# Probabilities and values split into high and low parts, the row maxima sent as one row by DMA, and the dense block's weights split inside it

## What is computed

```python
# attention: 2 x 8 heads, 768 positions, 64 values each
q_bits = (q @ proj > 0); k_bits = (k @ proj > 0)     # 6 bits each: a bucket
mask = bucket(q)[:, None] == bucket(k)[None, :]
scores = where(mask, q @ k.T / 8, -1e9)
scores = scores - max(scores, axis=-1)
attn = exp(scores); attn = attn / (sum(attn) + 1e-9)
x = attn @ v                                         # (1536, 512) over the heads
# dense block
h = x @ w_in; g = where(h > 0, h, exp(min(h, 0)) - 1); y = g @ w_out   # 512 -> 2048 -> 512
# experts: rows with y @ w_skip > 0 go through one of 8 experts, chosen by y @ w_gate
```

## Time and profile before

| what | value |
|---|---|
| median of three runs | 715.51 us |
| profiled execution, span | 718.39 us, 716.5 us |
| first scores of head 0, first `up` of the dense block | 24.6, 295.1 us |
| PE busy | 678.6 us, 95% |
| DVE, ACT, POOL busy | 326.7, 238.2, 192.9 us |
| attention matmuls of `weighted` (L1125) | 384 records, 152.8 us |
| moved by DMA | 83.95 MB, mean 117 GB/s |

### The profile page before, as it was taken

The page is one execution under the profiler, slowest core; times in us unless marked ns, Lnnn a source line. Parts: engine busy times, 40 slices in busy tenths (PEclk is TensorE's granted clock), DMA queues, the critical chain, the costliest instruction groups (busy, mean ns, idle before and its releaser), DMA issues.

```text
span 716.5 us, 9192 instructions
## 1 busy us (share of the span) xinstructions
PE 678.6 (95%) x3472; PEld 574.7 (80%) x3472; DVE 326.7 (46%) x475; ACT 238.2 (33%) x365; POOL 192.9 (27%) x179
## 2 busy tenths in 40 slices
PE   4999999998999999999999999999998975999996
PEld 3677767676777777799999989989997954989995
DVE  6766656565666654133232223222314257446542
ACT  1233334333333334333342334233422321334330
POOL 3322253535162430659120002000002034112111
PEclk9999999999999999999999999999999995999999
DMA  7456656564555530412020002000366765699200
GB/s 176 118 129 141 165 125 163 125 162 96 139 117 133 116 89 10 131 44 67 1 90 1 1 0 88 0 0 0 146 200 206 241 238 188 237 346 334 89 11 24
DMA packets 69235, 83.95 MB, mean 117 GB/s; under 512 B 35540, under 2 KB 45780, under 8 KB 69200
## 3 DMA queue, kind: packets, MB, share of 16 engines
q1 hardware_dynamic: 67920, 79.83, 38.1%
q0 software_dynamic: 1280, 3.65, 1.6%
HBM read 56.64 MB, written 8.44 MB: 91 GB/s over the span
## 4 chain that ended last, share of the span: by engine, by line
PE 85%; DMA 5%; DVE 4%; SPq 2%; ACT 1%; issue 1%; POOL 0%; POOLq 0%; DVEq 0%; ACTq 0%
PE banks L1179 18%; PE banks L1166 18%; PE banks L1125 15%; PE banks L1290 8%; PE banks L1305 6%; PE banks L1093 5%; DMA k_hi_lo_T<-qk_lo_T 4%; PE banks L1112 4%; PE banks L1113 4%; SPq L312 2%; PE banks L1077 2%; PE banks L1197 1%; DVE g_lo L839 1%; PE banks L1101 1%; DVE row_max L770 1%
## 5 line engine op out<-in xcount | busy, mean ns | idle before, releaser
L1125 PE MATMUL banks<-probs,v_ones 128*128 128x384 f32 x384 | 152.8, 490 | 0.3 <-ACT o_and_den L629 0.3
L1166 PE MATMUL banks<-x_hi,w_split 128*128 (+1 forms) x512 | 142.4, 339 | 0.8 <-DVE g L860 0.8
L1179 PE MATMUL banks<-w_split,g_hi 128*128 128x512 f32 x384 | 122.2, 399 | 4.8 <-DVE g_lo L839 4.8
L860 DVE SCALAR_TENSOR_TENSOR g<-exp_min_h,banks 128x384 f32<-128x384 f32 x64 | 35.5, 554 | 198.0 <-ACT exp_min_h L672 197.8
L645 ACT ACTIVATE probs<-banks 128x768 f32<-128x768 f32 x96 | 77.8, 811 | 132.3 <-PE banks L1113 132.3
L770 DVE TENSOR_REDUCE row_max<-banks 128x1 f32<-128x768 f32 x96 | 91.4, 957 | 66.5 <-PE banks L1093 64.7
L1166 PEld LDWEIGHTS banks<-x_hi,w_split 128*128 128x128 f32 x512 | 94.2, 189 | 4.0 <-DVE g L860 1.1
L669 ACT ACTIVATE exp_min_h<-banks 128x384 f32<-128x384 f32 x64 | 31.5, 492 | 181.5 <-PE banks L1166 181.5
L1166 PE MATMUL banks<-x_lo,w_split 128*128 (+1 forms) x256 | 86.3, 337 | 0.0
L1179 PEld LDWEIGHTS banks<-w_split,g_hi 128*128 128x128 f32 x384 | 71.3, 190 | 18.0 <-DVE g_lo L839 6.0
L1093 PE MATMUL banks<-k_hi_rows_T,q_hi_rows_T 96*128 96x384 f32 x192 | 76.8, 487 | 7.8 <-DMA k_hi_lo_T<-qk_lo_T 7.5
(11 more groups left out here) (155 smaller groups left out, 835.0 us busy)
## 6 DMA issues: line engine op xcount, KB each, us to landing
expert_w<-in_moe_w SPq DMA_DIRECT2D x32, 1024.0 KB, 5.3
w_raw<-in_moe_w_in SPq DMA_DIRECT2D x16, 256.0 KB, 3.5
w_raw<-in_moe_w_out SPq DMA_DIRECT2D x16, 256.0 KB, 3.7
qk_nat<-in_q SPq DMA_DIRECT2D x16, 192.0 KB, 4.1
qk_nat<-in_k SPq DMA_DIRECT2D x16, 192.0 KB, 4.3
v_nat<-in_v SPq DMA_DIRECT2D x16, 192.0 KB, 3.0
q_hi_rows_T<-qk_hi_T SPq DMA_DIRECT2D x16, 192.0 KB, 2.7
k_hi_rows_T<-qk_hi_T SPq DMA_DIRECT2D x16, 192.0 KB, 3.0
```

The source lines that it names most:

```text
L860: dve.scalar_tensor_tensor(gb[:, j % 2, :], e_neg[:, j % 2, :], -1.0, banks[:, j % 2, 0:BN], ALU.add, ALU.max).then_inc(s_["g_ready"], 1)
L1125: mm = pe.matmul(banks[:, 6 + b, 0:HALF], v_ones[h % 2][:, s, :], probs[:, n % 4, b * HALF:b * HALF + HALF], start=(s == 0), stop=(s == QT ...
L1166: mm = pe.matmul(banks[:, j % 2, 0:BN], w, x, start=(c == 0 and w is hi and x is x_hi), stop=(c == KC - 1 and w is lo))
L1179: mm = pe.matmul(banks[:, 2 + t, :], g, W[:, j, part, :], start=(j == 0 and i == 0), stop=(j == FT - 1 and i == 2))
```

## The change

- `weighted`: probabilities and values are split. ACT makes the high parts (`high_probs`, `high_of_v`), POOL all low parts (`low_probs`, 96 of 128 x 768, and `low_of_v`). Each half is three fp32r matmuls (of 386 columns in half 0: two columns of ones carry the sum of a row for the 1e-9) in place of one float32 matmul, and follows its scores by four steps (`LAG`) instead of two. The means of values are gone, with `VSUM`, `centre_v` and the addition in `normalise`.
- The minus maxima are 6 x 128 on DVE, and SP's `copy_minus_maxima` makes one row of 768 of them; the first scores of a head wait for it (`neg_copied`). The 1e-9 is added by ACT in `outputs`, with a small sum beside it.
- `head_units` is moved: `MAX` starts in step 0 of a head, `T` is in step 2, `MAX_T` in 3, `BITS` in 4. `outputs(h-1)` is in step 3. `inverse_den` is called after the second maximum of an odd head, and `normalise` one head later than before.
- SP: queries, keys and values of later heads are loaded first in a head, then `store_rden`, `load_w`, `load_rden`, then `copy_rows`, `copy_minus_maxima`, `copy_low_rows`.
- Four weight tiles are split during attention (heads 3, 5, 7, 9), twelve in the dense block's first pass by ACT (`high_of_w`) and DVE (`low_of_w`), two tiles ahead of use. The last three steps of `weighted` and the last `outputs` and `inverse_den` also lie in that pass.
- `split_x` is in halves; the first expert's weights are split in pieces, the second half after the first gather of rows. The buffers lie elsewhere in SBUF.

```diff
-EARLY = 9
+EARLY = 4
+LAG = 4
+RING = 4
@@ head_units
-    plan = [[], [("MAX", a, 0), ("MAX", a, 1)], [("MAX", a, 2), ("MAX", a, 3)],
-            [("MAX", a, 4), ("MAX", a, 5), ("T", b, 0)], [("VSUM", b, 0), ("MAX_T", a, 0)], [("BITS", b, 0)]][s]
+    plan = [[[], [("MAX", a, 0)], [("MAX", a, 1)]], [[], [("MAX", a, 2)], [("MAX", a, 3)]],
+            [[], [("MAX", a, 4)], [("MAX", a, 5), ("T", b, 0)]], [[], [], [("MAX_T", a, 0)]],
+            [[("BITS", b, 0)], [], []], [[], [], []]][s]
@@ SP
+            def copy_minus_maxima(h):
+                sp.wait_ge(s_["neg_done"], h + 1)
+                sp.dma_start(qb[h % 3][NEG_ROW:NEG_ROW + 1, :].bitcast(F32), neg[0:QT, h % 2, :].bitcast(F32))\
+                    .then_inc(s_["neg_copied"], 16)
             for h in range(HEADS):
+                if h + 3 < HEADS:
+                    load_qk(h + 3)
+                if h + 2 < HEADS:
+                    load_v(h + 2)
                 if h % 2 and h >= 3:
                     store_rden(h // 2 - 1)
+                    if h // 2 <= EARLY:
+                        load_w(h // 2 - 1)
+                    load_rden(h // 2 - 1)
+                if h + 2 < HEADS:
+                    copy_rows(h + 2)
                 if h + 1 < HEADS:
-                    load_mean(h + 1)
+                    copy_minus_maxima(h + 1)
+                if h + 2 < HEADS:
+                    copy_low_rows(h + 2)
                 if h % 2 == 0 and h:
                     load_den(h // 2 - 1)
@@ POOL
+            def low_probs(n):
+                pool.wait_ge(s_["p_hi_ready"], n + 1)
+                if n >= RING:
+                    pool.wait_ge(s_["pv_done"], n - RING + 1)
+                pool.tensor_tensor(p_lo[:, n % RING, :, 0:HALF], probs[:, n % RING, :].rearrange("p (b n) -> p b n", b=2),
+                                   p_hi[:, n % RING, :, 0:HALF].bitcast(F32), ALU.subtract)\
+                    .then_inc(s_["p_lo_pool"], 1)
@@ ACT, each head
+                    n = QT * h + s
+                    if s == 3 and h + 2 < HEADS:
                         round_qk(h + 2)
+                    exponential(n)
+                    if n:
+                        high_probs(n - 1)
+                    if s == 3 and h:
+                        outputs(h - 1)
+                    if s == 5 and 0 < h < HEADS - 1:
+                        high_of_v(h + 1)
@@ DVE, each head
                     for t in range(QT):
                         maximum(h + 1, t)
+                        if t == 1 and h % 2 and h >= 3:
+                            inverse_den(h // 2 - 1)
@@ PE
-                mm = pe.matmul(banks[:, 6 + b, 0:HALF], v_ones[h % 2][:, s, :], probs[:, n % 4, b * HALF:b * HALF + HALF],
-                               start=(s == 0), stop=(s == QT - 1))
+                pe.matmul(to, v_hi[h % 2][:, t, :], high, start=(t == 0), stop=False)
+                pe.matmul(to, v_hi[h % 2][:, t, :], low, start=False, stop=False)
+                mm = pe.matmul(to, v_lo[h % 2][:, t, :], high, start=False, stop=(t == QT - 1))
@@ dense block, first pass: ACT, then DVE
+                    if first and j == 2:
+                        outputs(HEADS - 1)
+                    if first and EARLY <= j + 2 < FT:
+                        high_of_w(j + 2)
...
+                    if first and EARLY <= j + 2 < FT:
+                        low_of_w(j + 2)
+                    if first and j == 4:
+                        inverse_den(PAIRS - 1)
```

More of the change, by code:

```diff
@@ L61 @@
     for _s in range(QT):
[L62 removed]
+        PSUM_ORDER += [("SCORES", _h, _s)] + sum(head_units(_h, _s), [])
 PSUM_AT = {x: n for n, x in enumerate(PSUM_ORDER)}
@@ L527, in _ @@
[L527 to L543 removed]
+                part = slice(n % 2 * HALF, n % 2 * HALF + BN)
@@ new lines, in split_x @@
+                for i in parts:
+                    x = XT[:, n // 2 * KC + 2 * i:n // 2 * KC + 2 * i + 2, part]
+                    high = xh[:, 1 - n % 2, 2 * i:2 * i + 2, :]
+                    pool.tensor_scalar(high, x, 1.0, 1.0, ALU.mult, ALU.mult).then_inc(s_["x_step"], 1)
+                    pool.wait_ge(s_["x_step"], 2 * n + i + 1)
+                    for c in range(2):
+                        at = (n // 2 * KC + 2 * i + c) * S + n % 2 * HALF
+                        low = pool.tensor_tensor(x_lo[:, at:at + BN], x[:, c, :], high[:, c, :].bitcast(F32), ALU.subtract)
+                    if i:
+                        low.then_inc(s_["x_ready"], 1)
@@ new lines, in _ @@
+            low_of_v(0)
+            low_of_v(1)
+            for h in range(HEADS):
+                if h:
+                    low_probs(QT * h - 2)
+                    low_probs(QT * h - 1)
+                low_probs(QT * h)
+                low_probs(QT * h + 1)
+                if h % 2 == 0 and h >= 4:
+                    normalise(h // 2 - 2, *low_ready(QT * h + 1))
+                if h % 2 and h >= 3 and h // 2 <= EARLY:
+                    split_w(h // 2 - 1)
+                if h in (11, 13):
+                    split_x(0, ((h - 11) // 2,))
+                low_probs(QT * h + 2)
+                low_probs(QT * h + 3)
+                if 0 < h < HEADS - 1:
+                    low_of_v(h + 1)
@@ L861, in block_body @@
                                              ALU.add, ALU.max).then_inc(s_["g_ready"], 1)
+                    if first and j == 1:
+                        dve.wait_ge(s_["pv_done"], QT * HEADS)
                     if j:
@@ L1208, in block_body @@
                     if first:
-                        pass
+                        for late in {0: (3,), 1: (2, 1)}.get(j, ()):
+                            weighted(QT * HEADS - late, 0)
+                            weighted(QT * HEADS - late, 1)
                     elif j == 2:
```

304 lines of the change are left out of this document (139 added, 165 removed).

## The result

| | before | changed |
|---|---|---|
| median of 4 runs | 715.19 us (714.37 to 722.57) | 752.58 us (748.21 to 754.43) |
| ratio, 95% interval | 1 | 1.049 (1.041 to 1.057) |
| span of the profiled execution | 716.5 us | 751.5 us |
| first `up` of the dense block | 295.1 | 330.1 |
| first product with the experts' weights | 603.5 | 639.3 |

The account below looks back on a forecast made before the run. PE bound the kernel before; after, the copied rows' road, held by the broadcast in six odd heads. Attention +14.4, `weighted` +3.15, lost wait -0.8, tile 9 +0.5: +17.2 us, 733 us at the median; 8-in-10 range 694 to 749.

Parts of the forecast that it names:

- PE's work and the regular head: Attention: PE's work falls from 16.7 to 14.5 us a head; the road of copied rows makes a regular head 15.5 us.
- GpSimd: Attention: 1.86 us per subtraction, 16.0 us a head at most, the excess over 15.5 made up in the long heads.
- The broadcast's issue: Odd heads from 3 on: the broadcast of inverse denominators is issued 7.9 us into the head.
- In flight: the failed step: Odd heads from 3 on: the broadcast is in flight for 10.2 us, from 7.9 to 18.1, with all seven copies behind it.
- Drain: Odd heads from 3 on: the copies end 4.0 us after the broadcast, within bounds of 2.8 and 6.8 us.
- Who waits: After odd heads from 3 on: the next MAX comes at 22.1 instead of 16.7 us, 5.4 us late, 5.9 with weights ahead.
- The clock: After each long wait in attention: PE's lowered clock costs 1.7 us, in a pair of heads of 38.6 us.
- The end of attention: Heads 14 and 15 to the dense block: 11.6, 11.2 and 1.05 us, first `up` at 309.5 against 295.1, +14.4 us.
- Dense block: First pass: +3.15 us of `weighted`, -0.8 of a lost wait, +0.5 (0 to 3) for weight tile 9 behind the last broadcast.
- Afterwards nothing moves: After the dense block's first pass: no change; the second gather's data come by 610.6 and are wanted at 613.3.
- Drains slowly: Rival: copies end 6.8 us after the broadcast instead of 4.0, +16.8 us, 750 us; chance 0.1.
- Not held: Rival: the broadcast does not hold the copies; heads average 15.8 us, 692 us, 3.3% faster; chance 0.18.

Follow-up runs that it names:

- a1: Changed kernel with the broadcast of inverse denominators issued as two transfers of 64 partitions, outermost dimension 64 instead of 2: 688.2 us.
- a2: Changed kernel with the single broadcast of inverse denominators issued behind the two low-row copies of its head: 690.9 us.
- c1: Changed kernel with SyncE waiting for the head's row of maxima to land before issuing the next queries, keys and values: 748.9 us.
- c2: Changed kernel with the broadcast as two transfers of 64 partitions, each with outermost dimension 2, so still on two engines: 760.3 us.
- c3: Changed kernel with the broadcast as two transfers of 64 partitions, each with outermost dimension 4, so on four engines: 735.8 us.
- a3: Changed kernel with the same single broadcast issued from ScalarE's queue instead of SyncE's: 740.4 us.
- b2: Kernel before with the broadcast as two transfers of 64 partitions and the first expert's weights split in pieces of 128x512: 703.0 us.

## Why the prediction was wrong

The direction and the main mechanism were right: six stalls in odd heads behind the broadcast, no long one elsewhere, and the time outside them close. The step that failed is "The broadcast is in flight from 7.9 to 18.1 (10.2 us)": with the copies queued on its two engines it is in flight for 12.7 to 14.7 us. A second step, who waits for the copies, was wrong too. The term that the forecast itself held to be weak, 4.0 us from its end to the last copy, measured 3.2 to 4.1. Step by step:

- **PE's work and the regular head.** `weighted` at 0.17 to 0.18 us a matmul, as forecast. No head between two stalls is free of the low clock: 4, 6, 8, 10 and 12 take 16.5 to 17.7 us, 17.1 in the mean, forecast 15.5 + 1.7 = 17.2; a1's from head 3 on take 15.4. Right, though `MAX` waits only once, 1.2 us. The first three heads took 3.1 us more than forecast (head 3's first scores at 72.4 against 69.3). (By its own terms PE's 14.5 is 14.7, and the 13.9 beside it 13.7; this moves the sum by 0.2 at most.)
- **GpSimd.** 1.69 us a subtraction instead of 1.86, 0.8 us of waits. No bound here.
- **The broadcast's issue.** Forecast 7.9 us into the head, by the earlier trace rows; it was 6.3 in head 11 and up to 7.3 in others, since denominators and store followed one another faster. That helped by 0.6 to 1.7.
- **In flight: the failed step.** Forecast 10.2 us, in heads 3 to 9 with 0.5 more for the weights. The 10.2 came from the earlier trace rows. There the copies were issued only from 194.26 on, 1.4 us before the broadcast ended, and for most of its flight it ran alone:

```profile
192.00:194.00 2.00, 2.00 (x15) 1.00 0.13 51
```

In the change they are issued from 2 to 3 us behind it on. The forecast queued them behind the broadcast and let them cost it nothing; measured, its flight was 2.5 to 4.0 us longer than forecast. a2 and c1 show the shares, 3.1 us for the copies and 0.6 for the loads; a1 (spread: hardly a wait), c2 (two engines: all of it), c3 and a3 (in between) show that it is the two engines. By what way transfers queued behind it slow the broadcast no run tells.
- **Drain.** Forecast 4.0 us to the last copy; 3.2 to 4.1. Right.
- **Who waits.** I let `MAX` wait, 1.2 us into the next head. It was the head's first `scores`: the row of maxima lies on six engines, two of them held, and lands only 0.6 to 0.8 us before the last copy, while the scores want it 1.2 us earlier. The working says that the row is held too, and then "the sum does not change": that was the error. In head 11 the terms that were off are -1.6 (issue), +2.8 (flight), -0.7 (row instead of last copy) and +1.3 (scores instead of `MAX`): 22.75 us instead of 20.9.
- **The clock.** It stood at 0.50 for 10.2 us each time, 3.6 to 5.7 of them with PE at work: 1.8 to 2.8 us lost, 2.3 in the mean, instead of 1.7, after longer waits. Together a pair of heads took 40.4 to 41.3 instead of 38.1 to 38.6: over the five pairs from head 3 to head 13 203.9 us against 192.5, +11.4, of which the heads with a broadcast make +12.1 and those between -0.7.
- **The end of attention.** From head 13 to the first `up` 53.8 us against 47.7: 2.2 for one more such head, and 3.9 in heads 14 and 15, of which single waits (`o_and_den` 1.6, `probs_lo` 0.8) that the forecast did not have are 2.4. 3.1 + 11.4 + 6.1 = 20.6 us: 330.1 against 309.5.
- **Dense block.** The last broadcast took 11.4 us instead of 10.2, and the load of weight tile 9 landed 1.4 us after its end, 37.2 us into the block instead of 34. The tile was late by 4.1 us, and the clock stood at 0.52 for 6.5 us behind it, 7 us in all where I took 0.5 and bounded it by 3: the same mis-sized hold. It is the difference between the changed kernel's 309.2 us from the first `up` to the experts and a1's 302.2.

```profile
370.97 0.66 PE L1233 MATMUL banks<-x_hi,w_split 128*128 128x384 f32 x1 [4.07 <-DVE w_split L906]
```
```profile
370.50:377.00 6.50, 6.03 (x18) 0.52 0.51 163
```

- **"Afterwards nothing moves"** was wrong the other way: the pieces of the first expert's split took away 4.8 us of waits and their low clock. The two errors nearly cancel: 309.2 us against 308.4 before, where I had 2.85 more.
- **The rivals.** "Drains slowly", 750 us with a chance of 0.1, came nearest, but by luck: the drain was not slow, and the loads behind, which it gave as its reason, cost 0.6 to 0.8 us a head (c1). What was long was the flight. "Not held", 692 us, was refuted as a forecast, but as a price it was good: with the hold removed a1 has 688.2. What the change is worth by itself shows in a1 against b2, the kernel before with the same cure and the same pieces: 688.2 to 703.0, ratios 0.962 and 0.977.

The range ended at 749 because a tenth was left out above, just where it fell.

## What to carry to other kernels

A broadcast whose outermost dimension is small is not a small transfer: it is a long one on two engines, and every later transfer that has a part on them waits, on either queue, and makes it longer still (10.0 us alone, 13.8 with copies and loads). Put the large dimension outermost, or issue it behind what is urgent, and price what stands behind it with the engines' pace under load, not alone. When two transfers share a counter, read a hold from the last one only; and before calling a section unmoved, look for engines that are stretched there by a neighbour's long instruction.

## What the runs showed of the hardware

- Replicating two rows of 3 KB over 64 partitions each, in two transfers with no copies behind (head 15): 10.8 us on two engines, 7.3 on four, 3.9 on sixteen. In one window each: 51 GB/s with two engines, 102 and then 54 with four, 258 with sixteen. No run explains the fall to 54.
- An engine moved 25 GB/s where two or, for 0.6 us, four were at work, and 13 in the mean while all sixteen worked (206 GB/s in all).
- A transfer's counter steps once about 1 us after the issue if it is on fewer than 16 engines, and then once per engine: two late steps for the broadcast, six for the row of six partitions, of which exactly two were held.
- SyncE's issues, 0.6 us otherwise, took up to 4.58 us (weights at 357.57; 4.54 for a keys load at 127.63) behind the broadcast on two engines; in a1 none there takes over 1.1. That the queue itself fills is my reading of it.
- A 0.55 us DVE operation with two inputs took 4.51 us beside a 4.57 us GpSimd subtraction, and 0.55 beside pieces of 1.3 us in most places (mean of all 64: 584 ns after, 742 before).
